# In every step of the attention, the masked unit is turned before the scores of the unit two ahead

## What is computed

```python
scores = scale * np.matmul(q, k.transpose(0, 1, 3, 2))
thresh = np.max(scores, axis=-1, keepdims=True) - tau
scores = np.where(scores >= thresh, scores, -1000000000.0)
attn = np.exp(scores - np.max(scores, axis=-1, keepdims=True))
attn = attn / (np.sum(attn, axis=-1, keepdims=True) + 1e-09)
out = np.matmul(attn, v)
# then, per batch: u = x + (relu(x.T @ w_tok1) @ w_tok2).T
# y = u + relu(u @ w_ch1) @ w_ch2
# h = relu(y @ w_in); out = (h * sigmoid(conv3(h))) @ w_out
```

## Time and profile before

| | |
|---|---|
| median of 3 runs | 893.38 us (892.24 to 894.54) |
| the profiled execution's own time | 894.54 us |
| its span, first to last instruction | 892.7 us |
| granted TensorE clock, mean | 0.992 |
| TensorE / VectorE / ScalarE / GpSimd busy | 95% / 48% / 46% / 31% |
| attention, roughly | the first 355 us |

### The profile page before, as it was taken

How to read it: one execution, slowest core, us unless ns; L and a number is a source line. 1 busy time by engine, 2 the same in 40 slices (tenths; PEclk the granted TensorE clock), 3 DMA queues, 4 the chain that set the end, 5 groups by cost and what they waited for, 6 DMA issues and landing times.

```text
span 892.7 us, 14832 instructions
## 1 busy us (share of the span) xinstructions
PE 847.3 (95%) x5544; PEld 665.0 (74%) x5544; DVE 429.5 (48%) x828; ACT 411.2 (46%) x866; POOL 278.4 (31%) x218
## 2 busy tenths in 40 slices
PE   7789989999999999889999999999999999999998
PEld 3456656666666666668888888888899989899996
DVE  5877767777777777271121121121121827437280
ACT  4577777777777777522111111121111737457371
POOL 0333333333333333252020020030075463618180
PEclk9799999999999999999999999999999999999999
DMA  9111111111111111400000000000040000010101
GB/s 270 51 50 47 49 48 48 47 47 47 47 47 47 47 48 16 142 1 1 1 1 0 1 1 1 0 1 1 5 161 25 2 23 26 1 59 0 47 0 59
DMA packets 20906, 33.75 MB, mean 38 GB/s; under 512 B 4416, under 2 KB 11136, under 8 KB 20864
## 3 DMA queue, kind: packets, MB, share of 16 engines
q1 hardware_dynamic: 20864, 33.18, 11.4%
HBM read 28.46 MB, written 4.72 MB: 37 GB/s over the span
## 4 chain that ended last, share of the span: by engine, by line
PE 88%; ACT 4%; issue 3%; DVE 2%; POOL 2%; ACTq 0%; POOLq 0%; DVEq 0%
PE score L1115 17%; PE score L1218 11%; PE score L974 6%; PE out_t L1130 4%; PE turn_y L1130 4%; PE mixed L1130 4%; PE tails L1130 4%; PE out_t L1030 4%; PE mixed L1073 4%; PE out_t L1203 4%; PE mixed L1030 4%; PE score L993 3%; PE turn_y L1203 2%; PE mixed L1203 2%; PE tails L1203 2%
## 5 line engine op out<-in xcount | busy, mean ns | idle before, releaser
L812 DVE TENSOR_SCALAR_CACHE_REDUCE negs<-score,neg_scale 128x576 f32<-128x576 f32 x144 | 112.7, 816 | 93.8 <-PE score L974 63.7
L890 DVE SCALAR_TENSOR_TENSOR h<-score,h 128x512 fp32r<-128x512 f32 (+1 forms) x60 | 38.3, 638 | 241.2 <-ACT h L677 241.2
L677 ACT ACTIVATE h<-score 128x512 fp32r<-128x512 f32 (+1 forms) x60 | 33.3, 555 | 255.3 <-PE score L1115 255.3
L829 DVE SCALAR_TENSOR_TENSOR prob<-negs,thresh,exps 128x576 f32<-128x576 f32 x144 | 140.6, 1009 | 0.3 <-ACT thresh L588 0.3
L585 ACT ACTIVATE exps<-negs,neg_max 128x576 f32<-128x576 f32 x144 | 104.9, 776 | 3.2 <-DVE negs L812 2.8
L1115 PE MATMUL score<-uh,w1h 128*128 128x512 f32 (+1 forms) x240 | 89.1, 371 | 3.2 <-DVE ul L860 3.2
L1115 PE MATMUL score<-uh,w1l 128*128 128x512 f32 (+1 forms) x240 | 89.0, 371 | 0.0
L1115 PE MATMUL score<-ul,w1h 128*128 128x512 f32 (+1 forms) x240 | 88.9, 370 | 0.0
L553 POOL TENSOR_TENSOR zl<-z,zh 128x512 fp32r<-128x512 f32 x32 | 54.8, 1711 | 98.7 <-ACT zh_t L751 98.7
L597 ACT ACTIVATE probT<-score 128x512 f32<-128x512 f32 x64 | 38.3, 598 | 80.2 <-PE turn_y L993 80.2
L974 PE MATMUL score<-qk 64*128 64x512 f32 x256 | 74.5, 659 | 0.0
(11 more groups left out here) (181 smaller groups left out, 2049.3 us busy)
## 6 DMA issues: line engine op xcount, KB each, us to landing
qk<-in_qk SPq DMA_DIRECT2D x16, 704.0 KB, 4.1
vm<-in_v SPq DMA_DIRECT2D x16, 320.0 KB, 4.3
result<-ostage SPq DMA_DIRECT2D x16, 256.0 KB, 2.1
w1f<-in_moe_w_ch SPq DMA_DIRECT2D x4, 768.0 KB, 10.7
w2f<-in_moe_w_ch SPq DMA_DIRECT2D x4, 768.0 KB, 7.0
wif<-in_moe_w_in SPq DMA_DIRECT2D x1, 2048.0 KB, 7.3
wof<-in_moe_w_out SPq DMA_DIRECT2D x8, 256.0 KB, 2.6
wt2f<-in_moe_w_tok SPq DMA_DIRECT2D x1, 576.0 KB, 10.0
```

Of the source, the lines that this page charges most:

```text
L812: nc.vector.tensor_scalar(negs[:, i, h, :], raw_of[h], neg_scale[:, 0:1], None, ALU.mult, ALU.min, accum_out=neg_max[:, i, h:h + 1]).then_ ...
L829: nc.vector.scalar_tensor_tensor(out=prob[:, i, h * S:(h + 1) * S], in0=negs[:, i, h, :], scalar=thresh[:, i, h:h + 1], in1=exps[i][:, h, ...
```

## The change

In each step the call that turns the masked unit s stands ahead of the call that computes the scores of unit s+2. All else stays in place, on all engines.

```diff
--- before.py
+++ after.py
@@ -1138,10 +1138,10 @@
                 g, k = at.g, at.k
                 for s in range(NT):
                     two, three = at.unit(s + 2), at.unit(s + 3)
+                    if at.units:
+                        turn_probs(at, s)
                     if two:
                         scores(two)
-                    if at.units:
-                        turn_probs(at, s)
                     if at.pv and s < 2:
                         times_v(g - 1, k - 1, (2 * s, 2 * s + 1))
                     if at.units and s < FULL:
```

## The result

The changed kernel takes 926.9 us (median of 4 runs, 926.33 to 927.72), the kernel before in the same runs 893.9: a ratio of 1.037, 95% interval 1.036 to 1.039. The forecast was 929, range 912 to 943.

A forecast was written before the change was run, and what follows sets the result against it. TensorE was taken to set the pace in the attention, with VectorE's work hidden under it. Loop 22, start 11 and clock 3 sum to 36 us on 893.4, forecast 929, range 912 to 943.

The forecast's parts named there:

- the start: Pairs 0 and 1, with less TensorE work to hide the ring: +11 us, plus 3 for an earlier, longer half clock.
- the ring: Cycle of copies, mask, second half of the turning, scores, copies: 3.2 us a step without masks.
- The pair: One pair of heads in the attention loop: period 24.2 us against 22.5, +1.7 in each of 13 pairs.
- The three ring steps: Units 2 to 3, 0 to 1 and 1 to 2, where the ring was to exceed TensorE's own work.
- The term of 22: Steady loop, pair 2 to pair 15: +1.7 us in each of 13 pairs, 22 us.
- The two masks: VectorE's masks of units 0 and 1 on the ring: m0 2.4 us behind GpSimd's xl, m1 1.56 running free.
- a fall of the clock after 60 us: Sign against the forecast: it would be wrong if the granted clock falls after 60 us.
- The waits of L993: Sign: transposes of L993 wait for the mask of L829 about once or twice a pair, 1 to 1.5 us each.
- masks as long as before: Rival, chance 0.18: GpSimd's work slides along with the ring, period 25.3 us, total 943.
- masks free: Rival, chance 0.15: masks run free, in the start too, and the clock holds; 12 plus 9 us, total 914.
- not slower: Rival, chance 0.05: turning first lets ScalarE drain sooner, h1l comes 0.5 us earlier in each of 13 pairs; total 887.
- The clock in the steady loop: Rival, chance 0.05: clock falls in the steady loop too, 2.5 us a pair, 33 us more, total 962.

The follow-up runs named there:

- the ring is cut: Changed kernel with VectorE's mask of unit s+1 moved ahead of its copies of unit s+2 in each step: 899.1 us, ratio 1.0061 against the kernel before.
- the zeros: Changed kernel plus two 512-column matmuls of zeros in each step of pair 0, ahead of the score tails: 921.8 us, ratio 1.0311 against the kernel before.
- step 3 alone: Kernel before, with transposes ahead of scores only in step 3 of pairs 2 to 15: 890.2 us, ratio 0.9957.

## Why the prediction was right

**The mechanism** held: the copies wait for scores, the scores for the turning, the turning for the mask, the mask for the copies. The loss is in the start and in steps 0, 1 and 4, and it goes when the ring is cut.

**The pair** was forecast at 24.2 and took 23.93 (24.07 as the mean of 13, with pair 2). By steps: 4.60 against 4.76, 5.19 against 5.1, 4.46 against 4.6, 3.88 against 4.05, 5.80 against 5.73. The three ring steps without their masks came out 0.1 to 0.2 short: half a turning after a stop does take 0.46, but the scores behind it only 0.91 to 0.93 instead of 1.06. The stop is not the reason, for the scores of unit 0 are as short behind a turning that never stopped, and unit 4's are longer than the 0.91 before:

```profile
223.85 1.06 PE score L976 x2
...
228.44 0.92 PE score L974 x4
```

I had taken the 1.06 from scores that stand right behind their tails. In the chains of both kernels it holds throughout the loop: scores of two heads take 1.06 behind tails and 0.91 to 0.93 behind the turning, unit 4's 0.91 and 1.06. Why is not shown. Over the three steps that is 0.42 a pair too many, 5.5 us in 13 pairs; the mask of unit 0, 0.16 longer than I had it, gives back 2. The term of 22 measured 18.7, and 1.4 of these are pair 2 at the lower clock, which was not in it: the ring by itself gave about 17.

**The two masks**: 2.56 (the chain at 234.98) and 1.55 (240.57 to 242.12), forecast 2.4 and 1.56. So unit 1's mask got away from GpSimd, as worked out, and unit 0's did not. The mask at 234.89 took 1.88 while xl ran from 234.61 to 236.17: about 1.1 of waiting and its own 0.8. It ended 0.60 after xl. The Trainium skill ("SBUF — State Buffer", Who interferes with whom) has the loser of the shared port blocked; this trace agrees nearly. By sharing the two masks would have summed to 4.6; they summed to 4.11, against 3.96 forecast. The 18.7 by itself decides less, since the short scores are in it.

**The start** was forecast at 11 for the ring and 3 for the clock; 13.3 were measured (14.3 from the first copies on, which start at 7.43 in the one trace and at 8.45 in the other), and the zeros took back 3.0 of them by pair 2, and 5 in all. The clock fell earlier than before, as forecast: it was granted 0.87 from 16 to 20 us and 0.50 from 20, with TensorE busy 2.42 of 4 us, no stop over 1.5 us, and nothing of GpSimd's split begun before 26.92. The argument, the half-busy stretch of the earlier trace rows, is weaker than it looks: the kernel before was busy 2.40 of 4 us from 16 to 20 and kept 1.00, and the kernel with only VectorE's order turned was busy 4.55 of 8 us from 16 to 24 and kept 1.00, where the changed kernel with 4.95 had 0.68. The Trainium skill ("TensorE: Matmul & The Clock Gate", Why this matters for your kernels), which ties the fall to idle gaps, would have put it only around that split; the trace decides against that reading here.

**What would have shown it wrong**: I had named a fall of the clock after 60 us. There was one, in pair 2 (0.67 from 64 to 72 us), not in the loop behind it; by this sign the forecast was wrong there, at a price of 1.4 us. The waits of L993 came 34 times in 12 pairs, nearly three a pair at 0.5 each, instead of one or two at 1 to 1.5, since TensorE has the first head's transposes between two shorter waits. That they are fewer and longer was a wrong reading of the same ring. The wait for h1l went away as forecast. **The rivals**: masks as long as before (943) was half true, for unit 0 alone; masks free (914) and not slower (887) were refuted by the same rows. The mechanism of the last is real, though: step 3 alone shows it, at -3.3 us, because there no mask is waited for. The clock in the steady loop (962) did not come in the changed kernel; it came in the kernel with only VectorE's order turned, in 8 of 13 pairs, at 0.7 us each instead of the 2.5 I had for it. The remark that the loop of the kernel before keeps full speed with a wait of 1.35 gave the mean wait; the longest is 2.2.

## What to carry to other kernels

Before an in-order engine's work is reordered, write down what the instruction moved ahead waits for, and what stands behind it: a wait that cost nothing behind independent work becomes a ring across engines when the work that feeds the waited-for engine is put behind it. Work out the ring for each step beside the engine's own work; the same edit may cost in one step and pay in the next, so it should be made step by step. And where a queue elsewhere (here ScalarE's drains and exponentials, VectorE's copies and masks) was laid out for the old order, test both orders of it.

## What the runs showed of the hardware that I had not expected

The granted clock fell in a stretch in which TensorE worked 2.42 of 4 us and stood still for 1.5 us at most, while the loop of the changed kernel, busy 21.42 of 23.93 us with one gap of 1.0, kept it full. The same stretch need not end the same way: behind a wait of 2.2 us for h1l in pair 4 the kernel before kept 1.00, and the kernel with only its start changed fell to 0.66 over 4 us. With only VectorE's order turned, such waits of 2.0 us led to a fall in 8 of 13 pairs. And a collision between a VectorE mask and a GpSimd split works both ways: xh (128x640) took 1.24 us beside a mask in the kernel before, and 0.72 in the changed kernel, where no mask runs at that time.
